# Attention into two gated feed-forward layers: the first batch's attention reordered in plain fp32, the last x block rounded later, w_out rounded a piece per step

## The reference

```
k_p, v_p = mean over 8 consecutive positions of k, v        # 576 -> 72 keys
scores = q @ k_p.T / 8;  attn = softmax(scores)             # per batch and head
x0 = attn @ v_p                                             # 8 batches x 576 tokens, 8 heads x 64
h  = x0 @ w1_in;  g = max(0.01 h, h);  x1 = g @ w1_out      # 512 -> 2048 -> 512
h  = x1 @ w2_in;  g = h * clip(h + 3, 0, 6) / 6;  out = g @ w2_out
```

## Time and profile before

| | us |
|---|---|
| median of 3 runs | 1704.76 (1704.0 to 1704.78) |
| the profiled execution | 1704.56 |
| its span | 1702.8 |

### The profile page before, as it was taken

How to read it: one execution, slowest core, us unless ns; L and a number is a source line. 1 busy time by engine, 2 the same in 40 slices (tenths; PEclk the granted TensorE clock), 3 DMA queues, 4 the chain that set the end, 5 groups by cost and what they waited for, 6 DMA issues and landing times. The chain is left out here.

```text
span 1702.8 us, 32933 instructions
## 1 busy us (share of the span) xinstructions
PE 1675.4 (98%) x10460; PEld 1489.4 (87%) x10460; DVE 1007.7 (59%) x1807; ACT 627.9 (37%) x1329; POOL 395.3 (23%) x427
## 2 busy tenths in 40 slices
PE   7999999999999999999999999999999999999999
PEld 6777888888888888888999888988989898989898
DVE  6767777676676867765455555444545454444444
ACT  4544433333333433333323333333333333333333
POOL 6226551021120212112432112121111212121200
PEclk8999999999999999999999999999999999999999
DMA  6745778768686786858787757666756675757562
GB/s 197 244 154 195 260 253 247 234 202 278 197 260 222 227 261 204 273 179 280 234 271 245 251 174 227 175 222 176 223 180 222 174 226 174 227 173 227 173 202 75
DMA packets 215810, 366.83 MB, mean 215 GB/s; under 512 B 22464, under 2 KB 47040, under 8 KB 215744
## 3 DMA queue, kind: packets, MB, share of 16 engines
q1 hardware_dynamic: 215744, 366.04, 68.1%
HBM read 308.28 MB, written 57.67 MB: 215 GB/s over the span
## 5 line engine op out<-in xcount | busy, mean ns | idle before, releaser
L1431 PE MATMUL ps_h<-xs_hi,ring 128*128 128x256 f32 x3808 | 814.8, 283 | 10.6 <-ACT p L1056 4.9
L1431 PEld LDWEIGHTS ps_h<-xs_hi,ring 128*128 128x128 f32 x3808 | 642.8, 189 | 56.4 <-issue 15.9
L1431 PE MATMUL ps_h<-xs_lo,ring 128*128 128x256 f32 x1904 | 534.3, 281 | 0.0
L1431 PEld LDWEIGHTS ps_h<-xs_lo,ring 128*128 128x128 f32 x1904 | 358.1, 188 | 25.7
L939 ACT ACTIVATE g_hi<-gate 128x512 fp32r<-128x512 f32 x288 | 181.9, 632 | 397.7 <-DVE gate L1137 212.7
L1384 PE MATMUL ps_y<-g_hi,wout_hi 128*128 128x512 f32 x576 | 225.7, 392 | 0.4 <-DVE y_stage L1192 0.4
L1386 PE MATMUL ps_y<-g_hi,wout_lo 128*128 128x512 f32 x576 | 225.4, 391 | 0.0
L1385 PE MATMUL ps_y<-g_lo,wout_hi 128*128 128x512 f32 x576 | 225.2, 391 | 0.0
L1196 DVE TENSOR_TENSOR u<-ps_h,p 128x256 f32<-128x256 f32 x272 | 114.3, 420 | 186.8 <-PE ps_h L1431 152.1
L1385 PE MATMUL ps_y<-wout_lo,g_hi 128*128 128x512 f32 x576 | 224.2, 389 | 0.0
L1386 PE MATMUL ps_y<-wout_hi,g_lo 128*128 128x512 f32 x576 | 224.2, 389 | 0.0
(11 more groups left out here) (115 smaller groups left out, 1994.2 us busy)
## 6 DMA issues: line engine op xcount, KB each, us to landing
ring<-w_in_split SPq DMA_DIRECT2D x920, 256.0 KB, 2.8
w_in_split<-ring SPq DMA_DIRECT2D x56, 256.0 KB, 3.5
w_in_split<-stage SPq DMA_DIRECT2D x56, 256.0 KB, 3.6
k_raw<-in_kT SPq DMA_DIRECT2D x32, 288.0 KB, 3.8
q_raw<-in_qT SPq DMA_DIRECT2D x32, 288.0 KB, 5.3
v_raw<-in_v SPq DMA_DIRECT2D x32, 288.0 KB
x0T<-x_stage SPq DMA_DIRECT2D x32, 288.0 KB, 3.8
x1T<-y_stage SPq DMA_DIRECT2D x36, 256.0 KB, 5.0
```

The costliest lines, as they stand in the source:

```text
L1431: mm = pe.matmul(banks[BANK_OF[r]], a, b[:, r, c, :], start=r in OPENS and c == 0 and n == 0, stop=c == 1 and n == 2, skip_group_check=True)
```

## The change

- Batch 0: the common list is replaced by one list per engine (`FIRST_DVE`, `FIRST_ACT`, `FIRST_PE`). `pv0`/`pv1` become one plain fp32 matmul per head (`v_f`, `pT_f`), so `turn_p*` loses DVE's rest and POOL's `v_hi`, `v_sum`, `v_lo` go. DVE sums the keys of all four pairs. Pair 3's second half uses pair 0's banks. PE's list holds the chunks of tile 0's step 0 (`upper`, `lower`), mixed with pair 3's attention. The counts and places of the warming matmuls change.
- Late tiles: `x_hi` of B22 moves from the last place of a tile behind the first `p1` copy of the next.
- w_out: ACT rounds pieces singly (after steps 5, 6 of T = 8 and 0 to 5 of T = 9), and DVE's places follow. SP's list is as it was.
- POOL: `v_lo(3, 0)` moves from ahead of the last `sums_lo` of tile 1 to behind `t_sums(2)`.

```diff
-LATE_X_HI_AT = (0, 1, 2, 3, 4, 5, 7)
-LATE_PIECE_AT = ((7, 6), (7, 7), (1, 6), (1, 7), (3, 6), (3, 7), (5, 6), (5, 7))
+LATE_X_HI_AT = (0, 1, 2, 3, 4, 5)
+LATE_PIECE_AT = ((6, 6), (7, 1), (1, 6), (2, 6), (3, 6), (4, 6), (5, 6), (6, 6))
...
+FIRST_DVE = [("sum_k", 0), ("sum_k", 1), ("scores", 0), ("scores", 1), ("sum_k", 2),
+             ("normalize", 0), ("divide", 0), ("scores", 2), ("sum_k", 3), ("normalize", 1),
+             ("divide", 1), ("scores", 3), ("normalize", 2), ("divide", 2), ("normalize", 3),
+             ("divide", 3), ("split_x", 0), ("split_x", 1), ("split_x", 2), ("split_x", 3)]
+FIRST_ACT = [("place_k", 0), ("place_k", 1), ("exp", 0), ("exp", 1), ("place_k", 2),
+             ("turn_p0", 0), ("exp", 2), ("pv0", 0), ("place_k", 3), ("round", 0),
+             ("turn_p1", 0), ("turn_p0", 1), ("pv1", 0), ("exp", 3), ("round", 1), ("pv0", 1),
+             ("turn_p1", 1), ("turn_p0", 2), ("split_x", 0), ("round", 2), ("pv1", 1),
+             ("pv0", 2), ("turn_p1", 2), ("turn_p0", 3), ("split_x", 1), ("pv1", 2),
+             ("turn_p1", 3), ("split_x", 2), ("pv0", 3), ("round", 3), ("pv1", 3),
+             ("split_x", 3), ("round", 4), ("round", 5), ("round", 6), ("round", 7)]
+FIRST_PE = [("scores", 0), ("scores", 1), ("scores", 2), ("turn_p0", 0), ("pv0", 0),
+            ("scores", 3), ("turn_p1", 0), ("pv1", 0), ("turn_p0", 1), ("pv0", 1),
+            ("turn_p1", 1), ("turn_p0", 2), ("pv1", 1), ("pv0", 2), ("turn_p1", 2),
+            ("turn_p0", 3), ("pv1", 2), ("turn_p1", 3), ("upper", 0), ("pv0", 3), ("upper", 1),
+            ("pv1", 3), ("upper", 2), ("lower", 0), ("lower", 1), ("lower", 2), ("upper", 3),
+            ("lower", 3)]
+WARM_STAGES = {("scores", 1): 4, ("scores", 2): 11, ("pv0", 0): 3, ("scores", 3): 5,
+               ("turn_p1", 0): 1, ("pv1", 0): 3, ("pv0", 1): 3, ("turn_p1", 1): 2,
+               ("pv0", 2): 2, ("turn_p1", 2): 2, ("pv1", 2): 1}
...
+        def half_buffers(b, c, half):
+            return units[0] if first(b) and c == PAIRS - 1 and half == 1 else buffers(b, c)
...
-            sum_k(2, 0)
-            sum_v(0, 2)
-            sum_k(3, 4)
-            sum_v(1, 6)
-            sum_v(2, 8)
-            sum_v(3, 10)
+            for c in range(PAIRS):
+                sum_v(c, 2 * c)
...
-                if i == HF - 1:
-                    v_lo(3, 0)
                 sums_lo(i)
...
             t_sums(2)
+            v_lo(3, 0)
...
                 nc.scalar.activation(p1[:], banks[0], ACT.Copy).then_inc(p1_ready, 1)
+                if i == 0 and last_x and not attention:
+                    x_hi(T, B22)
                 g_hi_of(s - 1, (i - 1) % HF, 0, before if i == 0 else layer)
...
                 step(TILES - 1, i, 1, prepares=[(7, 2 * HF)])
-                if i == HF - 2:
-                    piece_hi(PIECES)
-                    piece_hi(PIECES + 1)
+                if i in (HF - 3, HF - 2):
+                    piece_hi(PIECES + i - (HF - 3))
...
-                if i in (0, 2, 4):
-                    piece_hi(PIECES + i + 2)
-                    piece_hi(PIECES + i + 3)
+                if i < PIECES - 2:
+                    piece_hi(PIECES + 2 + i)
...
+                    if first(b):
+                        pe.wait_ge(pT_hi_ready, half + 2 * n + 1)
+                        for hd in range(2):
+                            mm = pe.matmul(at.ps[:, half, 0:n_q], u.v_f[:, hd, :],
+                                           at.pT_f[:, hd, 0:n_q], start=hd == 0,
+                                           stop=hd == 1)
```

More of the change, by code:

```diff
@@ L663, in _ @@
         def _(pool):
[L664 to L674, removed]
             def sum_v(c, folds):
@@ L1347, in _ @@
                 dve.memset(u.kT[:], 0.0).then_inc(kT_zeroed, 1)
-            for name, c in FIRST_STAGES:
-                if name != "round":
-                    stage(name, 0, c)
+            for name, c in FIRST_DVE:
+                stage(name, 0, c)
             for i in range(HF):
@@ L1474, in stage @@
                     half = int(name[-1])
+                    at = half_buffers(b, c, half)
                     pe.wait_ge(prob_ready, 2 * n + half + 1)
+                    if at is not u:
+                        pe.wait_ge(x0_copied, 2)
                     for hd in ((0, 1), (1, 0))[half]:
-                        if half == 1 and hd == 0:
+                        if half == 1 and hd == 0 and at is u:
                             pe.wait_ge(x0_copied, 2 * n + 1)
@@ L1482, in stage @@
                             mm = pe.transpose(
-                                u.ps[0:KEYS, hd, to:to + P - rows.start],
+                                at.ps[0:KEYS, hd, to:to + P - rows.start],
                                 u.prob[rows, SLOTS[half].start + 2 * j + hd, :],
@@ L1488, in stage @@
                     half = int(name[-1])
-                    pe.wait_ge(pT_ready, 2 * n + half + 1)
+                    at = half_buffers(b, c, half)
+                    n_q = PART_QUERIES[half]
                     if half == 0:
                         pe.wait_ge(v_ready, 2 * n + 2)
-                    for hd in range(2):
-                        n_q = PART_QUERIES[half]
-                        mm = product(u.ps[:, half, 0:n_q], (u.v_hi[:, hd, :], u.v_lo[:, hd, :]),
-                                     (u.pT_hi[:, hd, 0:n_q], u.pT_lo[:, hd, 0:n_q]),
-                                     hd == 0, hd == 1)
+                    if first(b):
+                        pe.wait_ge(pT_hi_ready, half + 2 * n + 1)
[3 more added lines that the diff above has]
+                                           stop=hd == 1)
+                    else:
+                        pe.wait_ge(pT_ready, 2 * n + half + 1)
+                        for hd in range(2):
+                            mm = product(u.ps[:, half, 0:n_q],
+                                         (u.v_hi[:, hd, :], u.v_lo[:, hd, :]),
+                                         (u.pT_hi[:, hd, 0:n_q], u.pT_lo[:, hd, 0:n_q]),
+                                         hd == 0, hd == 1)
                     mm.then_inc(pv_done, 1)
@@ L1507, in place @@
                         stage(name, 1, c)
+                if i == 0:
+                    for m in range(HF):
+                        place(m)
+                    return
                 first_part(i, 1, 0)
@@ L1574, in _ @@
             pe.wait_ge(zeroed, 2)
-            keep_warm(WARM_UP)
-            pe.wait_ge(v_zeroed, 2 * PAIRS)
+            keep_warm(WARM_UP, ps_y[:, DC - 1])
+            pe.wait_ge(v_zeroed, PAIRS + 2)
             pe.wait_ge(kT_zeroed, PAIRS)
-            for i, (name, c) in enumerate(FIRST_STAGES):
-                if name in ("scores", "turn_p0", "pv0", "turn_p1", "pv1"):
-                    if i < FIRST_STAGES.index(("place_k", PAIRS - 1)):
-                        keep_warm(WARM_STAGES.get((name, c), 2))
+            idle = ps_y[:, DC - 1]
+            for name, c in FIRST_PE:
+                if name in ("upper", "lower"):
+                    first_part(0, int(name == "upper"), c)
+                else:
+                    if (name, c) == ("turn_p1", 0):
+                        pe.wait_ge(shifted, 4)
+                        idle = ps_h[:, 0]
+                    if (name, c) == ("turn_p0", 1):
+                        idle = ps_att[:, 0]
+                    keep_warm(WARM_STAGES.get((name, c), 0), idle)
                     stage(name, 0, c)
```

57 lines of the change are left out of this document (25 added, 32 removed).

## The result

The changed kernel takes 1689.71 us (median of 4 runs, 1688.67 to 1690.43) against 1704.65 beside it (1704.0 to 1704.78): a ratio of 0.9909, 95% interval 0.9896 to 0.9921. It is 14.9 us faster; the prediction was 1688.4 (1684.0 to 1693.5), 16.35 less. The profiled execution took 1690.43, at the upper end of its runs (span 1688.6).

What follows compares the result with a forecast made beforehand. PE, busy 98% of the span, was taken to bound the kernel, so only closing its stalls or shortening its start pays. 7.5 + 1.25 + 3.4 + 4.2 = 16.35 us off 1704.76 gave 1688.4 us, range 1684.0 to 1693.5.

Steps and rivals of the forecast that it cites:

- 1. Batch 0: Start of the kernel: step 0 ends 11.3 us earlier, of which 7.5 us are left after a wait for batch 1's v.
- its lower end: Batch 0's gain if the load of batch 1's first v lands as late as 43 us: 5.5 us.
- rival (b): Clock falls in PE's 3.5 us wait at 44 us, costing 2.4 us more: 1690.8 us; chance 0.13.
- 2. Tile 1's sums: End of tile 1: PE's stall behind POOL goes, 1.25 us, bounds 0 to 2.3.
- 3. Pieces of w_out: T = 8 and 9: single pieces remove PE's waits behind DVE and ACT, 3.4 us, from 1.5 to 4.
- The 0.3 taken off for a collision: End of T = 8: DVE's piece at (7, 1) runs beside POOL, making `u3` late; 2.15 us becomes 1.85.
- 4. B22 behind `p1`: Eight late starts, T = 10 to 17: `p1` comes 0.52 us earlier at each, 4.2 us; bounds 3.2 and 4.6.
- Nothing takes its place: Late starts: no new wait replaces PE's removed one, so the full 0.52 us a start is gained.
- (a): Batch 1's first v arrives in time, so batch 0 brings 10.1 us instead of 7.5: 1685.8 us; chance 0.2.
- (c): Late starts do not gain, `p1` stays where it is and 4.2 us are lost: 1692.6 us; chance 0.07.
- (d): Batch 0's three engine lists wait for each other, leaving 3 us of 7.5: 1692.9 us; chance 0.07.
- (e): Slower: the low clock holds on through tile 0, PE's stream being broken up by waits for DVE: 1708.4 us; chance 0.03.

Runs made afterwards that it cites:

- e1: Changed kernel with SP issuing the load of batch 1's first v ahead of the three block stores instead of behind them: 1688.22 us.
- e2: Changed kernel with ACT rounding block A12 of step 0 right behind block 2, not after its copy of the last plain second product: 1687.05 us.
- e3: Changed kernel with 20 warming matmuls placed in PE's wait ahead of the first second product: 1688.61 us.
- e7: Changed kernel with POOL taking the rest of v's pair 3 ahead of tile 1's last sums again: 1690.87 us.
- e5: Changed kernel with the first rounding of x's block B22 back ahead of the `p1` copy: 1693.69 us.
- e9: Changed kernel with the edits of e1 and e2 together: 1686.43 us.
- e4: Changed kernel keeping the plain second product, but batch 0 in the old common order with few warming matmuls and step 0 behind the last pair: 1693.46 us.
- e11: e9 with DVE taking the rest of w_out's first piece ahead of batch 1's first maxima and subtractions: 1689.61 us.
- e8: Kernel before with the new batch 0 alone, the edits of e5, e6 and e7 together on the changed kernel: 1701.56 us, ratio 0.9973.
- e6: Changed kernel with w_out's pieces reloaded and rounded in pairs again: 1694.93 us.

## Why the prediction was right, point by point

**1. Batch 0: right in kind, too large by 3.25 in the profiled execution (7.5 against 4.25; six profiles give 4.25 to 6.32).** The chain of steps held, each a little late:
- Step 0 ends at 40.84, predicted 39.7 (the terms of that sum add up to 39.6). PE starts the scores of pair 3 at 18.25, 0.45 later than in my list. The plain product was priced right: four records from 23.80 to 25.16, 1.36 us, against 1.33.
- v was issued at 38.12, predicted 36.8. The reason is the one I gave, A12 behind ACT's copy of `pv0` 3 and then POOL's rest; e1 and e2 each take one link out of it and v comes early. It was used 5.1 us after its issue, against 4.2; in the six other profiles with this order of SP's list that is 4.0 to 4.5. The second product starts at 49.73, predicted 47.4: 5.3 us won, not 7.6. The prediction had this case as its lower end, 5.5 us if the load lands as late as 43; DVE used v at 43.23.
- So 2.3 of the shortfall are there at the second product. The rest, about 1, comes behind it, where the prediction lost nothing, and there the step that failed is rival (b), which I held at 0.13: the clock did fall. In e3, where it stays up, the 5.7 us won at the second product are 6.4 at the start of T = 1. I priced it at 2.4; e3 against the changed kernel and its repeat gives 1.8 to 2.4. "PE's work ahead of the wait is dense" was no protection. The earlier trace rows had shown the fall behind a single idle us of a PE already on and off, and a predicted wait of 3.5 us, found by my own sum, should have been taken as the likely case.

**2. Tile 1's sums: 2.0 instead of 1.25.** The stall of 1.11 went. So did the next one, 0.6 us at 250.13, which I had put into the bound (2.3) and not into the value. Step 7 of tile 1 takes 13.14 us in the kernel before and 13.13 in e7, but 11.08 in the changed kernel and 11.15 in its repeat.

**3. Pieces of w_out: 4.6 instead of 3.4.** The mechanism was right, three sizes were low. The gaps of before there are 2.33 behind DVE (2.15 less 0.3 in my sum), 1.79 behind `p1` (1.55), and 0.35 in small waits of step 1 that I had not counted: 4.5. The 0.3 taken off for a collision was not due. The piece moved to (7, 1) runs in 1.22 us although POOL takes up its first rest of x 0.22 us behind it; it is POOL's operation that takes longer, 2.16 us where its next one takes 1.30. So the 2.29 that I took for a piece beside POOL is not what every overlap costs:

```profile
921.29 1.22 DVE L1171 TENSOR_TENSOR wout_lo<-wout_raw,wout_hi 128x1024 fp32r<-128x1024 f32 x1
921.51 2.16 POOL L760 TENSOR_TENSOR xs_lo<-x_stage,xs_hi 128x512 fp32r<-128x512 f32 x1 [30.48 <-ACT xs_hi L915]
```

**4. B22 behind `p1`: 8 x 0.42 = 3.4 instead of 4.2**, a late tile 83.44 and not 83.35. PE's wait went as told. "Nothing takes its place" was wrong by 0.10 a start: I had looked at when POOL takes up B22's rest, and that did not move; what moved with `p1` is DVE's `gate`, into the time of the POOL rest ahead of B22's. e5 gives 3.1 for the part.

**The sum.** 4.25 + 2.0 + 4.6 + 3.4 = 14.25, where the column ends at 14.1 and the medians differ by 14.9. Terms 2 and 3 were too small by 1.95, 1 and 4 too large by 4.05, so that part of the agreement is luck. The terms leave out what belongs to none of them, 0.6 won in step 1 of tile 1 and 0.5 lost in T = 7. T = 7's steps 5 and 6 together take from 0.1 us less to 0.7 more than before in these profiles; no edit touches it, and its cause stays open.

**The other rivals.** (a) v in time: in e9 it is, and batch 0 then brings 8.76 and not 10.1, because DVE's list reaches the second product at 46.2 and not at my 44.9. (c), (d) and (e) did not happen; (d), engines that wait for each other, is what e4 shows of the old order.

## What to carry to other kernels

When a stage is pulled forward, list every transfer that an in-order queue issues behind something that was not pulled forward with it: here one block rounded late held a load of 288 KB, and with it a quarter to a half of the 8.8 us that the stage brings when the load is in time. A predicted wait of the matmul engine of the size found here, 3.4 us or more, should be priced with the low clock behind it: all six profiles with such a wait show it. Where a critical copy is made earlier, look at what its own followers on other engines then run beside.

## What the runs showed of the hardware that I had not expected

- The clock stayed at 1.00 behind waits of 1.47 us (e1, e9) and 2.03 (e11), and fell behind 1.92 (e2) and 3.4 to 4.7 (the changed kernel, its repeat and e5 to e8), each time with PE busy up to the wait; behind 4.71 it came back within 54 to 56. In the old order it fell at 32 to 33 us, near waits of only 1.1 to 1.6, with PE busy 1.5 (e4) and 1.75 (before) of the 3 us from 30 to 33. So the length of one wait does not decide it.
- It stayed low for 6.8 us in four of the profiles with that wait and for 3.4 in two (e6, e7), and the work behind it took 1.8 to 2.4 and 1.1 to 1.2 us longer than with the clock up (e3).
- A VectorE operation of two inputs in SBUF took 0.86 us when a GpSimd operation had 0.31 us to go as it started, and 1.39 when that had 0.84 to go (`gate` at the late starts, e5 and the changed kernel).
- A matmul in plain fp32 appears as two records; at the full clock the four records of 384 columns took 1.36 us (23.80 to 25.16) and those of 192 columns 0.65 (21.34 to 21.99), so it goes by columns down to there.
- The same batch 0 moved by 2 us from profile to profile; the time at the low clock moved by 3.4 us in it, and the landing of one load by 1.
